# Attention, MLP and soft mixture of experts in one program: another order of the beginning, and folds as two fp32r products

## What is computed

```python
# 1: attention, 4 batches x 8 heads x 768 positions x 64; windows of 32 queries,
#    keys from 16 before to 8 after the window, and 8 memory keys
scores = scale * np.matmul(q_c, k_full.transpose(0, 1, 3, 2))
scores = scores - np.max(scores, axis=-1, keepdims=True)
a = np.exp(scores)
a = a / (np.sum(a, axis=-1, keepdims=True) + 1e-09)
out[:, :, c_start:c_end] = np.matmul(a, v_full)
# 2: MLP, 3072 tokens, 512 -> 2048 -> 512
h = x @ w_in
g = h * (1.0 / (1.0 + np.exp(-h)))
x = g @ w_out
# 3: soft mixture, 8 experts x 4 slots
logits = x @ phi                       # softmax over tokens (d) and over slots (c)
slot_input = d.T @ x                   # 32 slots
h = np.maximum(slot_input[e] @ w1[e], 0.0); slot_out[e] = h @ w2[e]
return (c @ slot_out)
```

## Time and profile before

| | |
|---|---|
| median of 3 runs | 473.94 us (473.88 to 474.88) |
| the profiled execution | 473.49 us |
| its span, first to last instruction | 471.7 us |
| PE busy | 451.2 us (96%) |
| DVE, ACT, POOL busy | 274.4, 138.7, 45.3 us |
| chain that ended last | PE 85%, DMA 6%, DVE 4% |
| moved by DMA | 81.59 MB, mean 173 GB/s |
| mean granted clock of PE | 0.996 |

### The profile page before, as it was taken

One profiled execution on the slowest core, in us unless ns is written; L12 is line 12 of the kernel. 1 busy time (PEld: TensorE's weight loads), 2 busy tenths in 40 slices (PEclk: granted clock), 3 DMA queues, 4 the chain that ended last, 5 costly groups with the idle time before them and its releaser, 6 DMA issues.

```text
span 471.7 us, 12280 instructions
## 1 busy us (share of the span) xinstructions
PE 451.2 (96%) x5460; PEld 332.6 (71%) x5460; DVE 274.4 (58%) x532; ACT 138.7 (29%) x255; POOL 45.3 (10%) x43
## 2 busy tenths in 40 slices
PE   5899999999999999999999999999999999999982
PEld 5799667777876787767777777787677778643551
DVE  5657457765586566766665675568544566551233
ACT  2655233232331322323332323323222121210022
POOL 2476000000000000000000000000000000010000
PEclk9999999999999999999999999999999999999998
DMA  8979222321142153303331231130150479999997
GB/s 330 405 295 375 90 95 96 103 92 50 60 191 55 49 190 101 102 1 102 103 96 51 57 101 60 47 131 1 27 243 0 179 263 406 376 401 423 421 423 323
DMA packets 14308, 81.59 MB, mean 173 GB/s; under 512 B 1584, under 2 KB 1712, under 8 KB 7856
## 3 DMA queue, kind: packets, MB, share of 16 engines
q1 hardware_dynamic: 14256, 80.81, 45.4%
HBM read 74.51 MB, written 6.29 MB: 171 GB/s over the span
## 4 chain that ended last, share of the span: by engine, by line
PE 85%; DMA 6%; DVE 4%; ACT 1%; POOL 1%; issue 1%; DVEq 0%; POOLq 0%
PE h_ps L300 55%; PE o_ps L282 6%; DMA unit<-w 5%; PE lpu_ps L316 5%; PE lpu_ps L336 4%; PE sx_ps L259 3%; PE pt_ps L268 2%; PE sx_ps L336 2%; PE h_ps L964 1%; PE sx_ps L901 1%; POOL sc L776 1%; PE lpu_ps L324 1%; PE h_ps L901 1%; DMA qk_sb<-qk 1%; PE o_ps L944 1%
## 5 line engine op out<-in xcount | busy, mean ns | idle before, releaser
L300 PE MATMUL h_ps<-x_odd,wh 128*128 128x512 f32 x384 | 126.8, 400 | 0.0
L505 DVE SCALAR_TENSOR_TENSOR gT<-gT,h_ps 128x512 f32<-128x512 f32 (+1 forms) x108 | 66.4, 615 | 95.5 <-ACT gT L404 95.0
L404 ACT ACTIVATE gT<-h_ps 128x512 f32<-128x512 f32 (+1 forms) x108 | 58.6, 543 | 185.5 <-PE h_ps L300 184.5
L300 PEld LDWEIGHTS h_ps<-x_odd,wh 128*128 128x128 f32 x384 | 72.1, 188 | 21.4 <-issue 5.1
L300 PE MATMUL h_ps<-x_even,wh 128*128 128x512 f32 x256 | 85.0, 400 | 0.0
L300 PE MATMUL h_ps<-x_odd,wl 128*128 128x512 f32 x192 | 74.9, 390 | 0.0
L515 DVE STREAM_TRANSPOSE gB<-gT 128x512 f32<-128x512 f32 x80 | 56.7, 708 | 2.1 <-issue 0.3
L300 PEld LDWEIGHTS h_ps<-x_even,wh 128*128 128x128 f32 x256 | 48.0, 188 | 12.6 <-issue 2.2
L776 POOL TENSOR_TENSOR sc<-sc,row_stats 128x512 f32<-128x512 f32 x23 | 24.0, 1045 | 280.2 <-DVE row_stats L489 280.2
L300 PE MATMUL h_ps<-x_short,wh 128*128 128x256 f32 x256 | 50.6, 290 | 0.3 <-DVE x_short L494 0.3
L300 PE MATMUL h_ps<-x_even,wl 128*128 128x512 f32 x128 | 49.9, 390 | 0.0
(11 more groups left out here) (185 smaller groups left out, 495.4 us busy)
## 6 DMA issues: line engine op xcount, KB each, us to landing
unit<-w SPq DMA_DIRECT2D x31, 1024.0 KB, 9.3
qk_sb<-qk SPq DMA_DIRECT2D x24, 640.0 KB, 5.5
v_sb<-v SPq DMA_DIRECT2D x24, 512.0 KB, 3.6
out<-unit SPq DMA_DIRECT2D x6, 1024.0 KB, 7.4
w_stage<-w_in SPq DMA_DIRECT2D x4, 1024.0 KB, 8.0
wot<-w_outT SPq DMA_DIRECT2D x4, 1024.0 KB, 8.8
unit<-w_out SPq DMA_DIRECT2D x4, 1024.0 KB, 5.4
unit_acc<-w SPq DMA_DIRECT2D x1, 1024.0 KB, 10.2
```

Of the source, the lines that this page charges most:

```text
L300: last = nc.tensor.matmul(h_ps[k % 2][:, 0:TOKS[b]], w[:, n, kc, q * 128:(q + 1) * 128], x[:, lo, kc, 0:TOKS[b]], start=(kc == 0 and w is ...
L404: nc.scalar.activation(gt_of(b, k), h_ps[k % 2][:, 0:TOKS[b]], ACT.Tanh, scale=0.5).then_inc(tanh_done, 1)
L505: nc.vector.scalar_tensor_tensor(out=gt_of(b, k), in0=gt_of(b, k), scalar=1.0, in1=h_ps[k % 2][:, 0:TOKS[b]], op0=ALU.add, op1=ALU.mult).t ...
```

## The change

It touches the time before block 0, block 0 itself, and the folds of blocks 0 to 5.

- **Queue.** `w_in` 0 waits until `qk` 0 is in. `w_in` 3 stands ahead of `v` 3. `phi` and all four `w_outT` stand ahead of `qk` 4.
- **`w_in` by columns.** Halves of `wh` and `wl` are now 256 of 512 columns with all rows. PE waits for one half every second chunk, and POOL makes all eight low parts, where DVE had made one.
- **First scores.** PE scores unit 0 in two halves, and DVE takes each half's maximum apart. The sums of unit 0 stand ahead of unit 1. DVE normalises half of unit 1 beside POOL.
- **Block 0.** On PE scores stand ahead of values at the pause, on DVE `dve_scores` ahead of `dve_x`, and the sums ahead of `dve_g` of the next chunk; ACT's exponential comes one chunk earlier. `pe_w2` moves from chunk 13 to 9, its transpose from 14 to 10.
- **Folds.** In blocks 0 to 5 DVE writes `part_hi` (rounded to fp32r) and `part_lo` (the rest, one operation more), and PE makes two fp32r products with a rounded `fold_r` in place of one fp32 product. The last block keeps the old form.

```diff
             if b:
                 pe.wait_ge(acc_done, 4 * b)
-            nc.tensor.matmul(raw_ps(b)[:, 0:TOKS[b]], fold[:], part[:, 0:TOKS[b]], start=True, stop=True).then_inc(fold_mm, 1)
+            if b == LAST:
...
+            pe.wait_ge(fold_rounded, 1)
+            nc.tensor.matmul(raw_ps(b)[:, 0:TOKS[b]], fold_r[:], part_hi[:, 0:TOKS[b]], start=True, stop=False)
+            nc.tensor.matmul(raw_ps(b)[:, 0:TOKS[b]], fold_r[:], part_lo[:, 0:TOKS[b]], start=False, stop=True).then_inc(fold_mm, 1)
...
+                if b == 0 and at_pause:
+                    pe_scores(pe, scores_at(0, n))
                 if at_pause and values_at(b, n) is not None:
                     pe_values(pe, values_at(b, n))
...
+            nc.vector.tensor_copy(part_hi[:, 0:TOKS[b]], lg_ps(b)[:, 0:TOKS[b]]).then_inc(parthi_done, 1)
+            dve.wait_ge(parthi_done, b + 1)
+            if b:
+                dve.wait_ge(u_mm, b)
+            nc.vector.tensor_tensor(part_lo[:, 0:TOKS[b]], lg_ps(b)[:, 0:TOKS[b]], part_hi[:, 0:TOKS[b]].bitcast(fp32),
+                                    ALU.subtract).then_inc(part_done, 1)
...
             load_v(0)
+            sp.wait_ge(qk_in[0], 16)
             load_w_in(0)
...
             load_w_in(2)
+            load_w_in(3)
             load_v(3)
-            load_w_in(3)
-            load_qk(4)
-            load_v(4)
             sp.dma_start(phi_sb, phi).then_inc(phi_in, 16)
-            load_wot(0)
-            load_wot(1)
-            load_qk(5)
-            load_v(5)
-            load_wot(2)
-            load_wot(3)
-            load_qk(6)
-            load_v(6)
+            for n in range(NF):
+                load_wot(n)
+            for u in range(4, 7):
+                load_qk(u)
+                load_v(u)
```

More of the change, by code:

```diff
@@ L1 @@
+import itertools
 from contextlib import ExitStack
@@ L111, in moe_program @@
         eB = at("eB", 4096, [128, TMAX])
+        part_hi = at("part_hi", 3584, [128, TMAX], fp32r)
+        part_lo = at("part_lo", 4096, [128, TMAX], fp32r)
         stats = at("stats", 4608, [128, 8])
@@ L252, in pe_scores @@
                 pe.wait_ge(acc_done, 4 * dispatched - 1)
[L253 to L260, removed]
+            for ps in (range(0, 2), range(2, 4)) if u == 0 else (range(PAIRS),):
+                if ps[0]:
+                    last.then_inc(s_first, 1)
+                for t, c, p, h2 in itertools.product(range(2), range(2), ps, range(2)):
+                    a, r = place_of(p, h2)
+                    at = (2 * t + c) * WIN
+                    last = nc.tensor.matmul(s_of(u)[32 * r:32 * r + 32, a, at:at + WIN], q_of(u, t, c, p, h2),
+                                            k_of(u, t, c, p, h2), start=True, stop=True)
             last.then_inc(s_mm, 1)
@@ L290, in pe_mlp @@
                 pe.wait_ge(x_done, FIRST[b + 1])
[L291 to L294, removed]
+            if b == 0 and q % 2 == 0:
+                pe.wait_ge(wl_done, 2 * n + q // 2 + 1)
             if c >= 2:
@@ L323, in pe_fold @@
                 pe.wait_ge(acc_done, 4 * b)
-            nc.tensor.matmul(raw_ps(b)[:, 0:TOKS[b]], fold[:], part[:, 0:TOKS[b]], start=True, stop=True).then_inc(fold_mm, 1)
+            if b == LAST:
+                nc.tensor.matmul(raw_ps(b)[:, 0:TOKS[b]], fold[:], part[:, 0:TOKS[b]], start=True, stop=True).then_inc(fold_mm, 1)
+                return
+            pe.wait_ge(fold_rounded, 1)
+            nc.tensor.matmul(raw_ps(b)[:, 0:TOKS[b]], fold_r[:], part_hi[:, 0:TOKS[b]], start=True, stop=False)
+            nc.tensor.matmul(raw_ps(b)[:, 0:TOKS[b]], fold_r[:], part_lo[:, 0:TOKS[b]], start=False, stop=True).then_inc(fold_mm, 1)
         def pe_dispatch(pe, b, units_scored):
@@ L374, in pe_block @@
                     pe_logits(pe, b, n - 1)
-                if b == 0 and k == 13:
+                if b == 0 and k == 9:
                     pe_w2(pe)
-                if at_pause and scores_at(b, n) is not None:
+                if b and at_pause and scores_at(b, n) is not None:
                     pe_scores(pe, scores_at(b, n), b if k > dispatch_step(b) else 0)
-                if b == 0 and k == 14:
+                if b == 0 and k == 10:
                     pe_w2_T(pe)
@@ L461, in act_block, with dve_first_scores @@
                     act_dispatch(act, b - 1)
-                if k % 4 == pause(b) + (b == 0) and scores_at(b, n) is not None:
+                if at_pause and scores_at(b, n) is not None:
                     act_exp(act, scores_at(b, n))
+        def dve_first_scores(dve):
+            maxima = rmax[:, 0, :].rearrange("p (a g) -> p a g", a=2)
+            for a, scored in enumerate((s_first, s_mm)):
+                dve.wait_ge(scored, 1)
+                nc.vector.memset(sx_ps[:, a, 0:LEFT], NEG).then_inc(edge_first, 1)
+                dve.wait_ge(edge_first, a + 1)
+                nc.vector.tensor_reduce(maxima[:, a, :], by_window(0)[:, a, :, :], AX.X, ALU.max).then_inc(max_first, 1)
+            dve.wait_ge(max_first, 2)
+            nc.vector.tensor_tensor(sc_of(0), by_window(0), maxima.unsqueeze(3).to_broadcast([128, 2, 4, WIN]),
+                                    ALU.subtract).then_inc(sc_done, 1)
         def dve_scores(dve, u):
@@ L572, in dve_block @@
                 n, at_pause = k // 4, k % 4 == pause(b)
-                if b and k % 4 == pause(b) + 1 and scores_at(b, n) is not None:
+                if k % 4 == pause(b) + 1 and scores_at(b, n) is not None:
                     dve_sums(dve, scores_at(b, n))
@@ L782, in _ @@
         def _(act):
+            act.wait_ge(const_set, 5)
+            nc.scalar.copy(fold_r[:], fold[:]).then_inc(fold_rounded, 1)
             act_exp(act, 0)
```

59 lines of the change are left out of this document (34 added, 25 removed).

## The result

| | before | after |
|---|---|---|
| median of 8 runs each | 473.88 us | 475.90 us (475.21 to 476.91) |
| ratio, 95% interval | | 1.0047 (1.0035 to 1.0058) |
| the profiled execution, its span | 473.49, 471.7 us | 475.21, 473.2 us |
| PE busy | 451.2 us | 451.7 us |
| mean granted clock of PE | 0.996 | 0.986 |

The account below looks back on a forecast made before the run. PE was taken to bound blocks 1 to 5, waits block 0, weight loads the end. +4.85 + 1.4 - 0.9 - 2.2 = +3.15; 473.49 + 3.15 + 0.45 = 477.1 us, own range 474.9 to 479.7, with rivals 471.5 to 480.

Parts of the forecast that it names:

- What bounds the kernel: Whole kernel: PE bounds blocks 1 to 5, weight loads the end; gains or losses of folds and block 0 arrive there.
- The start: Before block 0: sums of unit 0 come first, so the chain from there moves 1.25 us earlier, bounds 0.7 and 1.5.
- PE at unit 4: Block 0: PE would reach the scores of unit 4 at 31.8 us, where values of unit 3 had started at 34.16.
- The load of unit 4 is not there: Block 0: qk 4 lands at 39.0 us behind phi and the w_outT, so PE waits from 31.8; +4.85 us.
- The clock: Block 0, behind the wait at unit 4: PE's clock falls and slows its products; +1.4 us, upper bound 1.85.
- The rest of block 0: Later block 0: waits of 0.41, 0.60 and 0.75 go, waits for gT come (+0.85); -0.9 us.
- The folds: Blocks 0 to 5: two fp32r products replace a 0.88 us fold, DVE's added operation mostly covered; -2.2 us.
- The load is there after all: Rival, block 0: qk 4 lands before 31.8 us and the wait vanishes; -5.5, 468.4 us; chance 0.08.
- the queue is quicker: Rival, block 0: qk 4 is in at 35.5 us, a 3.7 us wait spares the clock; 472.2 us; chance 0.12.
- they cancel: Rival: landing at 37.4 and no loss by the clock; +0.15, 474.1 us, no change; chance 0.14.
- DVE late in the blocks: Rival on top of the forecast: the low part adds 0.7 to DVE in five blocks; 478.9 or 480.6 us; chance 0.08.
- the signs named: Changed profile: PE idles 5.5 to 9 us before unit 4, clock falls, first chunk 1.25 us earlier, short gT waits.

Follow-up runs that it names:

- E1: The changed kernel with its loads from w_in 3 on in the order of before (qk 4 ahead of phi and w_outT), w2c still at chunk 9; 475.96 us.
- E4: The kernel before with only the folds of blocks 0 to 5 made as two fp32r products; 471.80 us, ratio 0.9964.
- E7: The changed kernel with qk 4 issued ahead of phi and v 4 left behind the four w_outT; 467.56 us, ratio 0.9868.
- E5: The kernel before with only the order of its loads changed, w_in 0 not waiting for qk 0; 477.21 us, ratio 1.0079.
- E3: The changed kernel with 28 fp32 products that nothing reads put ahead of the scores of unit 4; 474.19 us, ratio 1.0013.

## Why the prediction was right

It named the mechanism, the place and the sign, and the runs bear it out. Its sizes were off in both directions, which cancelled in part; that the total came within 1.2 us of the measured one owes something to that luck.

- **What bounds the kernel.** Right: what block 0 lost and the folds won arrived at the end. Between the last dispatch and the end of the span lie 63.4 us before and 62.45 after, but 62.6 to 64.3 in E1 to E4, whose code there is the same. So 0.95 us of the difference between the two profiled executions is the scatter of the weights' last landings, about the spread of the runs.
- **The start**, -1.25. Measured -0.59 (the first chunk at 18.42 instead of 19.01). Unit 0's chain was shortened as said, though by 0.83 only (POOL began `sc` at 9.67), for PE scored unit 0 more slowly. But the first chunk needs unit 1 too, and DVE came to unit 1's sums at 12.27 instead of 10.27, behind those of unit 0 and the copy of `pt`. PE then waited 0.84 for half of unit 1, where before it had waited 0.80 for `pt`:

```profile
4.71 1.54 PE L266 MATMUL sx_ps<-qk_sb 64*32 64x64 f32 x64 [0.20 <-DMA qk_sb<-qk]
...
7.33 1.18 PE L266 MATMUL lpu_ps<-qk_sb 64*32 64x64 f32 x64
...
14.38 0.66 PE L277 MATMUL pt_ps<-ident,sc_first 128*128 128x128 f32 x4 [0.84 <-POOL sc_first L521]
```

  1.54 stands against 1.18 in the earlier trace rows. Each product takes 0.31 us in both; with the heads in two halves their starts lie further apart, which no run took apart.
- **PE at unit 4.** 31.8 forecast, 31.93 measured, and 31.64 and 31.70 in E1 and E7. Three errors met. The start gave 0.66 less. The new wait for `gT` before chunk 5 came, but as a step of 0.26 at 28.08 instead of 0.4, too short for the list. And a wait for `sc` was worth more than its bracket: before, the transpose of unit 3 began 0.69 after the last product of the chunk (31.45 to 32.14), now 0.12 after it (29.78 to 29.90), so the bracket of 0.41 cost 0.57, and in the same way that of 1.14 cost 1.30.
- **The load of unit 4 is not there**, +4.85. Right in kind, shown by E5 (the order of the loads alone makes 3.3 us and the wait for `qk` 4), E1 and E7 (without it the wait is gone). The landing came at 38.1 instead of 39.0. The step that was mis-sized is `phi`: 1.35 us was read from a stretch before which the queue had run dry. Here `v` 3 landed at 17.05 + 9.4 = 26.45 and `phi` at 17.42 + 9.2 = 26.6, so it cost 0.2; the payload ahead of it came 0.45 later than the 26.0 of the sum. The rest, 11.5 us for four tiles and `qk` 4, is within 0.1 of the 4 x 2.5 + 1.6 of the sum. The estimate from the Trainium skill's ceiling in "DMA: Bandwidth & Descriptors", 34.5 us, was 3.6 too early: the queue moved 366 GB/s from 2.5 to 10 us and 415 from 10 to 38. Term by this landing: 38.14 + 1.87 - 36.03 = +3.98.
- **The clock**, +1.4. Too small by 0.9: scores and values took 41.15 - 38.14 = 3.01 us instead of 1.87, and chunk 7 about 2.7 instead of 1.5, 2.3 in all; E3 gave 2.0 back. I had taken 1.85 as the upper bound from the kernel's start, where the first group of scores is slow and the second, at 7.00, already fast. Behind the wait the low level lasted from before 38 until near 44. The bound did not even hold at the changed kernel's own start: there the second group, at 7.33, still took 1.18 (row above). PEclk reads 1.00 in that stretch all the same, so at the start the lengths of the products are the better witness.
- **The rest of block 0**, -0.9. Measured 4.48 - 3.98 - 2.3 = -1.8. The three waits went, and by the steps between products they had cost 0.57, 0.76 and 0.82, 2.15 instead of the 1.75 of their brackets; PE waited once for `gT`, a bracket of 0.20 and a step of 0.36, where +0.85 was allowed (the slow clock hides the wait before chunk 9, as the prediction said of a part of it; E3 has it as 0.26). 0.36 - 2.15 is -1.8, so nothing is left over.
- **The folds**, -2.2. Measured -2.0: block 0's gave 0.21, the next three 0.45 or 0.46 each, block 4's 0.37. Block 5's gave almost nothing (2.49 at the fold, 2.47 at the dispatch). E4 gives 2.0 by itself. DVE's added operation was covered: PE waited only 0.2 us between 62 and 395, as in the earlier trace rows, and in block 2 the raw logits were kept at 144.09 with the dispatch at 144.92, a margin of 0.83 where 0.65 was forecast.

**Sum.** +3.98 + 2.3 - 1.8 - 2.0 = +2.5 at the last dispatch, and the tail's -0.95 leaves +1.5 in the span, which is what the profiled executions show; +3.15 had been forecast. Three slips in the prediction's own numbers changed nothing: the upper end of its range, with both errors at once, is 479.45 and not 479.7; the payload up to `qk` 4 is 13.8 MB, not 13.9; and a margin of 0.3 us would still cover DVE's work, so the price of the last rival doesn't follow from it.

**The rivals.** *The load is there after all* falls by the 6.2 us of wait, *the queue is quicker* by the landing at 38.1 and the clock, *they cancel* mostly by the clock (the landing at 38.1 was 0.7 behind its 37.4), *DVE late in the blocks* by the 0.2 us of waits. What no rival held is that the same change with `qk` 4 ahead of `phi` and the weights would have won 6.3 us. Of the signs named, three were off: the first chunk was 0.59 and not 1.25 us earlier, the load landed 17.7 and not 19 us after its issue, and a wait for `gT` long enough for the list came once.

## What to carry to other kernels

When large transfers are pulled ahead on a queue, list what now stands behind them and when it is wanted: here 4 MB that PE comes to at 38.8 us passed 640 KB that it comes to at 31.7. Two moves that lean on each other (weights early, their product early) must be undone or kept together, as E1 shows. A long wait of TensorE can cost itself and then the clock, here 6.21 us and 2.3 more; products that nothing reads, in the place of the wait, gave 1.7 back. And the idle time in a bracket is less than a wait's price: here 0.41 stood for 0.57.

## What the hardware showed that was not expected

- PE's program comes in packets of 16 KB (256 instructions) through the DMA engines that carry the data. A packet lasts 0.9 to 1.1 us in the table above, PE goes on 2.2 to 2.5 us after it began, and where it began late PE stood for up to 2.7 us with no semaphore to show for it.
- The queue after it had run dry. In E1 nothing was issued between `qk` 4 at 17.82 and `v` 4 at 25.11, and from 25.5 to 26 the queue moved 92 GB/s. The windows behind it:

```profile
26.00:28.00 2.00, 2.00 (x18) 1.93 (x17) 1.93 (x6) 1.50 (x3) 0.12 (x1) 1.00 0.97 292
28.00:30.00 2.00, 2.00 (x17) 1.86 (x16) 1.40 (x4) 1.51 (x4) 2.00 (x2) 1.00 0.72 220
30.00:32.00 2.00, 2.00 (x51) 1.87 (x50) 0.87 (x2) 1.68 (x4) 2.00 (x2) 1.00 0.87 279
```

  220 to 292 GB/s, where the changed kernel, whose queue was never empty, moves 397 to 415 in 32 to 38 us. `phi`, with its small rows, lies in that stretch; which of the two slows it was not tried.
- The granted clock fell behind a wait of 3.49 us in E5's profiled execution, though by their mean clocks not in all of its runs, and read 1.00 for the first 4 us of the 6.21 us in the changed kernel.
